# Fewer unread identity products on TensorE in the first four steps of the attention

## The reference

```python
f = 1.0 / (1.0 + np.exp(-f_logit))
for t in range(S):
    state = f[:, :, t, :, None] * state + np.einsum('bhd,bhe->bhde', k[:, :, t], v[:, :, t])
    y[:, :, t] = np.einsum('bhd,bhde->bhe', q[:, :, t], state)
```

## Time and profile before

| | us |
|---|---|
| median of 3 runs | 822.7 |
| lowest and highest | 821.97, 823.2 |
| the profiled execution | 822.24 |
| its span | 820.4 |
| TensorE busy in the span | 785.2 (96%) |
| VectorE | 456.7 (56%) |
| ScalarE | 465.2 (57%) |
| GpSimd | 531.0 (65%) |

### The profile page before, as it was taken

The page is one execution under the profiler, slowest core; times in us unless marked ns, Lnnn a source line. Parts: engine busy times, 40 slices in busy tenths (PEclk is TensorE's granted clock), DMA queues, the critical chain, the costliest instruction groups (busy, mean ns, idle before and its releaser), DMA issues.

```text
span 820.4 us, 17851 instructions
## 1 busy us (share of the span) xinstructions
PE 785.2 (96%) x6053; PEld 749.6 (91%) x6053; DVE 456.7 (56%) x1136; ACT 465.2 (57%) x980; POOL 531.0 (65%) x500
## 2 busy tenths in 40 slices
PE   8999997299999999999999999999999999999995
PEld 8888886298999999999999999999999999999995
DVE  6799998794565476357635863585365622330001
ACT  5687775252675277428742873377347735853653
POOL 8788882668765368537852885288528854954652
PEclk9999999589999999999999999999999999999998
DMA  6666684130040041004100400040004004000000
GB/s 184 204 206 203 203 311 156 47 146 1 11 174 2 29 155 30 2 30 154 30 12 19 165 20 28 3 166 19 31 8 167 11 30 154 29 2 30 1 1 29
DMA packets 33740, 65.68 MB, mean 80 GB/s; under 512 B 4561, under 2 KB 20945, under 8 KB 33281
## 3 DMA queue, kind: packets, MB, share of 16 engines
q1 hardware_dynamic: 27072, 50.36, 18.3%
q0 software_dynamic: 3136, 9.64, 3.6%
q10 hardware_dynamic: 3456, 4.72, 1.6%
HBM read 55.26 MB, written 9.44 MB: 79 GB/s over the span
## 4 chain that ended last, share of the span: by engine, by line
PE 89%; DVE 4%; POOL 4%; issue 2%; ACT 1%; DVEq 0%; POOLq 0%; ACTq 0%
PE o_ps L1470 8%; PE o_ps L1472 8%; PE o_ps L1471 8%; PE m_ps L1450 6%; PE m_ps L1454 6%; PE m_ps L1458 6%; PE a_ps L640 3%; PE o_ps L1410 3%; PE m_ps L1392 3%; PE y_ps L607 3%; PE o_ps L1412 3%; PE m_ps L1390 3%; PE o_ps L1411 3%; PE m_ps L1393 3%; PE xr_ps L583 2%; PE y_ps L597 2%
## 5 line engine op out<-in xcount | busy, mean ns | idle before, releaser
L1091 POOL TENSOR_TENSOR t_lo<-whole,t_hi 128x384 fp32r<-128x384 f32 x190 | 211.4, 1114 | 86.3 <-ACT t_hi L1176 84.5
L1119 POOL TENSOR_TENSOR whole<-whole,below 128x384 f32<-128x384 f32 x126 | 137.9, 1094 | 131.2 <-ACT below L1195 130.3
L1470 PE MATMUL o_ps<-w_out_hi,t_hi 128*128 128x384 f32 x378 | 127.7, 338 | 0.9 <-POOL t_lo L1091 0.8
L1472 PE MATMUL o_ps<-w_out_hi,t_lo 128*128 128x384 f32 x378 | 126.6, 335 | 0.0
L1471 PE MATMUL o_ps<-w_out_low,t_hi 128*128 128x384 f32 x378 | 126.4, 334 | 0.0
L1450 PE MATMUL m_ps<-y_hi,w_in_hi 128*128 128x384 f32 x288 | 99.7, 346 | 0.0
L1454 PE MATMUL m_ps<-y_hi,w_in_low 128*128 128x384 f32 x288 | 96.6, 335 | 0.0
L1191 ACT ACTIVATE whole<-m_ps 128x384 f32<-128x384 f32 x96 | 47.0, 490 | 64.7 <-PE m_ps L1458 62.1
L1175 ACT ACTIVATE whole<-m_ps 128x384 f32<-128x384 f32 x48 | 23.6, 492 | 94.6 <-PE m_ps L1390 81.1
L1195 ACT ACTIVATE below<-below 128x384 f32<-128x384 f32 x128 | 67.3, 526 | 16.8 <-ACT below L1192 0.8
L1470 PEld LDWEIGHTS o_ps<-w_out_hi,t_hi 128*128 128x128 f32 x378 | 71.0, 188 | 2.2 <-issue 1.7
(11 more groups left out here) (278 smaller groups left out, 1896.6 us busy)
## 6 DMA issues: line engine op xcount, KB each, us to landing
w_raw<-w SPq DMA_DIRECT2D x16, 1536.0 KB, 6.5
f_in<-f_t SPq DMA_DIRECT2D x48, 96.0 KB, 2.3
k_in<-k_t SPq DMA_DIRECT2D x48, 96.0 KB, 2.3
q_in<-q_t SPq DMA_DIRECT2D x48, 96.0 KB, 2.3
v_in<-v_rows SPq DMA_DIRECT2D x24, 192.0 KB, 2.5
x_scratch<-x_row ACTq DMA_DIRECT2D x24, 192.0 KB, 2.5
w_in_raw<-w_in SPq DMA_DIRECT2D x1, 3072.0 KB, 12.3
w_out_raw<-w_out SPq DMA_DIRECT2D x1, 3072.0 KB, 21.0
```

The source lines that it names most:

```text
L1091: nc.gpsimd.tensor_tensor(t_lo[n % RING][:], whole[n % 3][:], t_hi[n % RING][:], ALU.subtract).then_inc(lo_made, 1)
L1119: nc.gpsimd.tensor_tensor(tile[:], tile[:], below[m % 2][:], ALU.subtract).then_inc(g_made, 1)
L1470: nc.tensor.matmul(o_ps[t][:], hi[:, rows], w_out_hi[:, m, :], start=(m == 0), stop=False)
L1472: ins = nc.tensor.matmul(o_ps[t][:], lo[:, rows], w_out_hi[:, m, :], start=False, stop=(m == MI - 1))
```

## The change

The numbers of products in the four calls of `keep_awake` become smaller: 18 to 11 in front of the first step, 26 to 16 in step 2 (behind the turning of tile 0's keys), 6 to 4 in step 3 ahead of the first scores, and 18 to 5 in step 3 behind them. The calls stay where they are.

```diff
                 if s in (2, 3):
-                    keep_awake(26 if s == 2 else 6)
+                    keep_awake(16 if s == 2 else 4)
                 if 3 <= s:
                     pb, c = at(b, o, 3)
                     scores(pb, c, s == 3)
                 if s == 3:
-                    keep_awake(18)
+                    keep_awake(5)
 
-            keep_awake(18)
+            keep_awake(11)
             run_steps(pe, step, tiles + 2)
```

## The result

| | before | after |
|---|---|---|
| median of 6 runs each, same chip | 822.95 us | 818.78 us |
| lowest and highest | 821.97, 823.63 | 818.4, 820.44 |
| profiled execution | 822.24 | 818.85 |
| its span | 820.4 | 816.9 |

The ratio is 0.9955 with a 95% interval of 0.9945 to 0.9965: faster by 0.45%. The forecast was 818.8.

The account below looks back on a forecast made before the run. TensorE's queue was taken as the bound, with unread identity products ahead of the attention's work. Removing 3.66 us gave 818.6 from the profiled 822.24 and 819.0 from the median 822.7; forecast 818.8, range 817.6 to 821.0.

Parts of the forecast that it names:

- The replay of the four steps: First 24 us, batch by batch with traced durations: line 607 starts at 18.48 instead of 22.14 us, 3.66 us earlier.
- What is late next: Ahead of line 607 after the cuts: VectorE's chain is late next, so removing more products would give nothing.
- Itself hung on the load of f_in: VectorE's chain ahead of the first mask was said to depend on the load of f_in; no size given.
- Does the shift survive: Attention behind the first line 607: other engines keep up, so all 3.66 us are taken.
- 0.2 us of lead come back in each step: Attention rounds: VectorE needs 4.85 us without waits against TensorE's 5.08, so it regains 0.2 us of lead each step.
- 4.85: VectorE's attention round without waits, in us: 3.56 from near to the mask plus 1.29 for the mask.
- the 0.3 to 0.7 kept for it: Allowance in us for the attention rounds: what is lost if VectorE's lead over TensorE fails.
- The clock: Thinner product cover from 14.9 to 18.35 us: the clock was taken to stay up, at no cost.
- the thin stretch: TensorE from 14.9 to 18.35 us, ahead of line 607: busy 1.8 of 3.4 us, put at 51%.
- the row with 63%: Window of the earlier trace with TensorE busy 1.89 of 3.0 us, where the clock stayed at 2.4 GHz.
- one fall: Rival: the clock falls once ahead of the attention's stream, costing 1.7 to 3 us; time 820.2 to 821.7; chance 0.14.
- The slower rival: From about 17 us the clock falls and the attention's own products don't raise it; time over 900 us; chance 0.04.

Follow-up runs that it names:

- run 1: The kernel before with only the fourth number of products cut (18, 26, 6, then 5 instead of 18): 819.85 us against 822.28.
- run 2: The kernel before with only the first three numbers cut (11, 16, 4), the last staying 18: 819.95 us against 822.28.
- run 8: The kernel before with three VectorE memsets (1.1 us) added ahead of the first mask: 823.07 us against 822.87.
- run 5: The changed kernel without the first batch of products, the others kept (16, 4, 5): 818.66 us against 822.29 for the kernel before.
- run 10: The changed kernel with the turned keys of tile 2 moved ahead of line 607 in step 4: 818.73 us against 822.87 for the kernel before.
- run 6: The changed kernel with the loads of f_in of tile 2 issued ahead of q and v of tile 1: 818.32 us against 822.29 for the kernel before.
- run 7: The changed kernel with three VectorE memsets (1.1 us) added ahead of the first mask: 824.36 us against 822.29 for the kernel before.
- run 4: The changed kernel with only the first batch of 11 products, then 0, 0, 0: 821.18 us against 822.28 for the kernel before.
- run 3: The changed kernel with no products at all: 822.11 us against 822.28 for the kernel before, times in two groups, 819.7 to 820.6 and 823.6 to 824.6.
- run 12: The changed kernel with no products, run once more for its spread: 819.95, 819.97, 820.25 and 824.27 us.
- run 9: The changed kernel with its pauses filled, 11, 19, 6, 10 products instead of 11, 16, 4, 5: 818.74 us against 822.87 for the kernel before.
- run 11: The changed kernel with f_in of tile 2 loaded earlier and, in steps 1 to 3, ScalarE's Exp ahead of growth: 817.57 us against 822.29 before.

## Why the prediction was right

*That the products are in front of the attention's work* held: runs 1 and 2 show the queue, and run 8 that a later mask costs nothing behind it.

*The replay of the four steps.* Predicted and measured: keys at 7.6 and 7.73, keys of tile 1 at 12.55 and 12.67, scores 14.5 and 14.71, mask 17.06 and 16.97 without a wait, line 607 at 18.48 and 18.35. The first batch took 5.06 us instead of 4.7: in this execution the clock came up later, at about 9 us, the products of the second batch still running cold for their first half microsecond. Nothing came of it, as run 5 explains: up to a microsecond of lateness there ends in a pause.

*What is late next* was named rightly, VectorE, and only just rightly at its root. "Itself hung on the load of f_in" is true by 0.1 us: the load ends last in the changed kernel's chain, and in run 10 its 0.56 us of lateness came through in full. As advice it failed, in run 6: the loop of k_s, Ln, growth, Exp, near and scan sets the pace 0.1 us behind it. The prediction had the rows to see it: k_s of tile 1 ended at 12.19 and Ln could not have started sooner, whatever e_x did.

*Does the shift survive.* Near of tile 3 at 23.6 and the third mask at 27.1 were forecast; 23.47 and 26.95 were measured, without a wait, where the earlier trace rows has 0.32. One row held to be fixed moved without harm: e_x of tile 4 came at 18.67 and not at 19.73, its load asked for at 15.52 instead of 16.50. "0.2 us of lead come back in each step" failed: these are the masks of the next rounds, and one k_s between them.

```profile
26.95 1.28 DVE L490 TENSOR_TENSOR a_m<-a_ps,causal 128x512 f32<-128x512 f32 x2
...
30.64 0.69 DVE L527 TENSOR_TENSOR k_s<-k_in,rb 128x512 f32<-128x512 f32 x1 [0.24 <-DVE rb L520]
...
31.92 1.28 DVE L490 TENSOR_TENSOR a_m<-a_ps,causal 128x512 f32<-128x512 f32 x2
...
36.93 1.28 DVE L490 TENSOR_TENSOR a_m<-a_ps,causal 128x512 f32<-128x512 f32 x2
...
46.12 1.29 DVE L490 TENSOR_TENSOR a_m<-a_ps,causal 128x512 f32<-128x512 f32 x2 [0.20 <-PE a_ps L640]
```

The rounds are 4.97 and 5.01 us, not 4.85, and VectorE waits for TensorE again only at 46. In both of them k_s waits 0.23 to 0.24 us for VectorE's own rb, which the round of the earlier trace rows that gave the 4.85 does not have, though the kernel before has it in its next two rounds. That cost 0.11 us (3.79 to 3.68), inside the 0.3 to 0.7 kept for it. Run 10 is the same fact from the other side.

*The clock.* That it would stay up held in the profiled execution: windows of the kernel after, as in the earlier trace rows.

```profile
14.90:18.30 3.40, 2.28 (x26) 1.00 0.71 201
...
8.00:134.00 126.00, 121.31 (x1735) 1.00 0.72 228
```

The share of the thin stretch was 2.28 of 3.40, 67%, not 51% (the prediction's own 1.8 of 3.4 is 53%): each group's last matmul is counted to its end, and the products ran 1.38 us by the timeline and not 1.1. It is on the side of the row with 63% that had stayed. Run 7 had the same share and fell, so the share ahead of the pause did not decide it. The chance of 0.14 for one fall was no exaggeration: run 7 has a fall with one longer pause, run 4 one with fewer products, and the 820.44 among the changed kernel's six times lies where that rival put its own. Its price was put at 1.7 to 3 us. The traces show 1.1 (run 7) and 1.7 (run 3) at the attention's end; the medians are 2.4 (run 4) and 3.3 (run 3) over the changed kernel, where time outside the span (run 4) and the upper group of executions (run 3) come on top. Of the 3.4 to 6 us of low clock from which the price was worked out no row gives the bounds, only the 4.9 us of the search that lie between; measured under the attention's stream were some 3 us (run 7) and 4 (run 4). The section of the Trainium skill that spoke against the change (TensorE: Matmul & The Clock Gate, "A second HAM failure mode", in which frequent short pauses between groups of matmuls make the gate swing, in a kernel that cycled through PSUM's banks) does not describe the changed kernel's profile, whose matmuls ran at full speed from 9 us to the attention's end, nor any other profile here: where the clock fell in the attention it fell in one pause and came back once.

*Where luck helped.* The profiled executions differ by 3.39 us: the 3.79 of line 607, less 0.11 in the VectorE rounds, 0.2 in the search and 0.1 outside the span. The medians differ by 4.17, since the kernel before took 822.95 beside the changed one and not the 822.7 of the forecast. That 818.8 met 818.78 to 0.02 us is luck. The allowance for the difference, half of the 0.5 us between median and profile, came out right; that the later rise of the clock is its cause was argued, and no run shows it.

*Two readings that were off*, without weight for the sum. The clock row is low in two slices, those of 144 to 185 us, and in the last, not in four. And the old stream had no pause in its first 19 us to set beside the four: from 2.73 to 22.14 TensorE was busy without a break.

## What to carry to other kernels

Price removed filler not by its own length but by the distance to the next thing that becomes ready, one wait at a time: here 7.2 us of products were worth 3.7, and two halves of the cut, worth 2.8 and 2.2, did not add. Products that hold the clock were worth having here only in the 10 us ahead of the full stream: enough to keep its last pause short, and none that stand in the queue when the stream's first input is ready. Where filler has been cut to the edge, look at what a small delay elsewhere would do, since the filler was also its cover.

## What the runs showed of the hardware

- The attention's own stream, about three quarters of its time in that stretch products of 48 rows or 48 columns and the rest turned keys of 112, raises TensorE's granted clock by itself: low at 18.4 to 22 us, 1.00 from 23 us on (run 4). The slower rival rested on the opposite.
- The same work in the 3.40 us ahead of 18.3 (2.28 and 2.30 us busy) went with a kept clock where the pause behind was 1.17 us, and with a fall where it was 2.43 us (run 7). The low level lasted from 19.0 to 22.5 us there.
- Without enough products, or with the longer pause, equal executions of one kernel differ by some 4 us in two groups (runs 3, 4, 7 and 12), the upper one with some 9 us more at half the clock in runs 4 and 7 by my estimate; the changed kernel's six lie within 2.0 us and those of runs 5, 6, 9 and 11 within 0.6.
